# A fused attention and mixture-of-experts kernel: the scores of a later step move to between the two halves of the value mix on TensorE

## What is computed

```python
scores = scale * np.matmul(q, k.transpose(0, 1, 3, 2))
mask = (rel >= 0) & (rel < window)
scores = np.where(mask, scores + bias[None], -1000000000.0)
scores = scores - np.max(scores, axis=-1, keepdims=True)
attn = np.exp(scores)
attn = attn / (np.sum(attn, axis=-1, keepdims=True) + 1e-09)
x = np.matmul(attn, v)            # then reshaped to (2304, 512)
expert_idx = np.argmax(x @ w_gate, axis=1)
h = np.maximum(np.einsum('ecd,edf->ecf', disp, w1), 0.0)
y = np.einsum('ecf,efd->ecd', h, w2)
```

## Time and profile before

| what | value |
|---|---|
| median of 3 runs | 388.81 us (388.73 to 388.84) |
| the profiled execution, its own time | 388.75 us |
| span of the profile | 387.0 us |
| what lies around the span | 1.75 us |
| attention in the profile | about 11.4 to 135.8 us |
| TensorE busy | 370.0 us, 96% of the span |
| mean granted TensorE clock | 0.992 of full speed |

### The profile page before, as it was taken

One profiled execution on the slowest core, in us unless ns is written; L12 is line 12 of the kernel. 1 busy time (PEld: TensorE's weight loads), 2 busy tenths in 40 slices (PEclk: granted clock), 3 DMA queues, 4 the chain that ended last, 5 costly groups with the idle time before them and its releaser, 6 DMA issues.

```text
span 387.0 us, 8491 instructions
## 1 busy us (share of the span) xinstructions
PE 370.0 (96%) x2978; PEld 318.8 (82%) x2978; DVE 252.1 (65%) x798; ACT 202.2 (52%) x535; POOL 145.1 (37%) x192
## 2 busy tenths in 40 slices
PE   7999999998999998999999999999999999999990
PEld 6787778876877677989989989988989998989980
DVE  6788677799978763767966547556777775542120
ACT  2978878887777612664635424444637644411100
POOL 7558989945643342423042043034033240011011
PEclk9999999999999999999999999999999999999996
DMA  8999999999851111687687365664776666001001
GB/s 163 202 320 204 226 227 232 256 257 218 187 85 56 55 29 56 205 256 257 197 268 229 117 200 179 171 180 169 241 257 232 191 221 209 2 28 45 3 25 51
DMA packets 81326, 64.90 MB, mean 168 GB/s; under 512 B 63982, under 2 KB 63982, under 8 KB 81264
## 3 DMA queue, kind: packets, MB, share of 16 engines
q1 hardware_dynamic: 73600, 52.19, 51.0%
q0 software_dynamic: 3840, 11.03, 8.6%
q10 hardware_dynamic: 3824, 0.80, 1.2%
HBM read 54.56 MB, written 11.02 MB: 169 GB/s over the span
## 4 chain that ended last, share of the span: by engine, by line
PE 78%; POOL 10%; DVE 5%; issue 2%; DMA 2%; ACT 1%; SPq 1%; DVEq 0%; POOLq 0%
PE ps L1485 59%; PE ps L1343 4%; PE ps L1316 4%; POOL weights_sb L617 4%; PE ps L1354 3%; PE ps L1282 2%; PE ps L1478 2%; PE ps L1324 2%; DMA q_rows<-in_q 2%; POOL probsT L624 2%; POOL v_step L605 2%; POOL weights_sb L616 2%; DVE ps L907 1%; DVE probs L920 1%; PE ps L1400 0%
## 5 line engine op out<-in xcount | busy, mean ns | idle before, releaser
L1485 PE MATMUL ps<-weights_sb,hiddenT 128*128 128x512 f32 x480 | 118.5, 393 | 0.0
L1485 PE MATMUL ps<-rowsT_hi,weights_sb 128*128 128x256 f32 (+2 forms) x512 | 115.0, 303 | 1.0 <-DVE rowsT_lo L1163 1.0
L1485 PEld LDWEIGHTS ps<-weights_sb,hiddenT 128*128 128x128 f32 x480 | 87.6, 188 | 16.6 <-DVE hiddenT L1182 0.2
L857 ACT ACTIVATE hiddenT<-ps 128x384 fp32r<-128x384 f32 (+1 forms) x64 | 30.6, 478 | 111.8 <-PE ps L1485 111.6
L1485 PEld LDWEIGHTS ps<-rowsT_hi,weights_sb 128*128 128x128 f32 x512 | 85.8, 188 | 2.6 <-issue 1.4
L1190 DVE TENSOR_TENSOR weights_sb<-raw,weights_sb 128x1024 fp32r<-128x1024 f32 x56 | 68.4, 1222 | 17.1 <-ACT weights_sb L845 16.9
L1485 PE MATMUL ps<-rowsT_lo,weights_sb 128*128 128x256 f32 (+2 forms) x256 | 76.7, 300 | 0.0
L1182 DVE SCALAR_TENSOR_TENSOR hiddenT<-ps,hiddenT 128x384 fp32r<-128x384 f32 (+1 forms) x64 | 34.5, 539 | 56.0 <-ACT hiddenT L857 55.8
L845 ACT ACTIVATE weights_sb<-raw 128x1024 fp32r<-128x1024 f32 x56 | 58.9, 1052 | 0.0
L682 POOL DMA_INDIRECT gathered<-x_rows,src_row x21 | 23.1, 1098 | 91.9 <-DVE weight_now L1176 87.3
L743 ACT ACTIVATE probs<-probs,mins 128x128 f32<-128x128 f32 x144 | 55.6, 392 | 0.6 <-DVE mins L920 0.4
(11 more groups left out here) (175 smaller groups left out, 489.0 us busy)
## 6 DMA issues: line engine op xcount, KB each, us to landing
raw<-in_moe_w SPq DMA_DIRECT2D x64, 512.0 KB, 4.7
q_rows<-in_q SPq DMA_DIRECT2D x16, 256.0 KB, 5.9
v_rows<-in_v SPq DMA_DIRECT2D x16, 256.0 KB, 5.4
x_rows<-x_sb SPq DMA_DIRECT2D x16, 256.0 KB, 4.9
k_rows<-in_k SPq DMA_DIRECT2D x14, 256.0 KB, 6.3
k_rows<-in_k ACTq DMA_DIRECT2D x2, 256.0 KB, 7.0
v_rows<-in_v SPq DMA_DIRECT2D x4, 128.0 KB, 5.8
v_front<-in_v SPq DMA_DIRECT2D x4, 128.0 KB, 6.2
```

The costliest lines, as they stand in the source:

```text
L857: nc.scalar.activation(hiddenT[0][c % RINGED][:, 0:P * size], hiddenT_ps(c, P * size), ACT.Relu).then_inc(hiddenT_hi, 1)
L1485: ins = te.matmul(dst, left[a], right[c], start=first and n == 0, stop=last and n == 2)
```

## The change

`mix` gets a parameter for the half that it does. In a step, the first half (values as loaded) is issued before `score`, and the second half (differences) after it. The waits go with the halves: `v_landed` and `probsT_whole` ahead of the first, `v_stepped` and `probsT_later` ahead of the second. The waits for `first_kept` and `early_kept` move ahead of the first half, and so ahead of `score`. The first two steps of the first span keep their order. In the two steps that have no score left to issue nothing is moved. No instruction is added or taken away, and the queues of the other engines stay as they are.

```diff
-            def mix(b, kk):
+            def mix(b, kk, part):
 
                 i, quad = divmod(kk, 2)
                 u = b * TI + i
-                values = [v_rows[:, u % RING, :]] + ([v_step[:, u % 2, :]] if i > 0 else [])
-                if quad == 0:
-                    pe.wait_ge(v_landed[u % RING], landed(u))
-                pe.wait_ge(probsT_whole, b * STEPS + kk + 1)
...
+                final = part == (1 if i > 0 else 0)
+                if part == 0:
+                    if quad == 0:
+                        pe.wait_ge(v_landed[u % RING], landed(u))
+                    pe.wait_ge(probsT_whole, b * STEPS + kk + 1)
+                    left = v_rows[:, u % RING, :]
+                else:
+                    pe.wait_ge(v_stepped, b * (TI - 1) + i)
+                    pe.wait_ge(probsT_later, b * (STEPS - 2) + kk - 1)
+                    left = v_step[:, u % 2, :]
+                for n in range(2):
+                    for odd in range(2):
+                        h = head(quad, 2 * odd + n)
+                        last = te.matmul(mixT_ps[DH * odd:DH * odd + DH, n, :], left[:, DH * h:DH * h + DH],
+                                         probsT[:, part, 2 * odd + n, :], start=(part == 0), stop=final)
+                if final:
+                    last.then_inc(mixed, 1)
...
+                    if last and kk == FIRST_INVERTED:
+                        pe.wait_ge(first_kept, 1)
+                    if last and kk in (4, FIRST_ROUTED[1] + 4):
+                        pe.wait_ge(early_kept, 1 if kk == 4 else 3)
+                    if not first or i > 0:
+                        mix(b, kk, 0)
                     if not (last and kk + 2 >= STEPS):
                         if not first or kk >= 2:
                             pe.wait_ge(back_kept, b * STEPS + kk - 1)
                         score(b + (kk + 2) // STEPS, (kk + 2) % STEPS)
-                    if last and kk == FIRST_INVERTED:
-                        pe.wait_ge(first_kept, 1)
-                    if last and kk in (4, FIRST_ROUTED[1] + 4):
-                        pe.wait_ge(early_kept, 1 if kk == 4 else 3)
-                    mix(b, kk)
+                    if first and i == 0:
+                        mix(b, kk, 0)
+                    if i > 0:
+                        mix(b, kk, 1)
```

## The result

The changed kernel takes 403.26 us (median of 4 runs, 402.98 to 404.03) and the kernel before 388.77 us (4 runs, 388.71 to 388.84) on the same chip. The ratio is 1.0372, with a 95% interval of 1.036 to 1.0384: slower. The forecast was 401.6 us, in a range of 397.0 to 405.5. The profiled execution took 403.5 us, its span is 401.8.

A forecast was written before the change was run, and what follows sets the result against it. TensorE's queue bounds the kernel (busy 370.0 of 387.0 us). Terms: 7.5 - 1.4 + 0.6 + 2.35 + 3.7 = 12.8 us, so 388.75 + 12.8 = 401.55, stated as 401.6 us; range 397 to 405.5.

The forecast's parts named there:

- The wait on GpSimd: Second half of the mix waits for GpSimd's `keep_later` in six steps; the change gains all 1.4 us.
- The stall for ScalarE's copy: Between `turn_back` and first half, TensorE waits for the probabilities' copy: 0.32 us (0.27 to 0.41) in 32 steps.
- The extra change of tile shape: Halves of the mix split by the score cost 0.15 us more a step, in 30 steps; bounds 0 and 0.34.
- The rival in which it is free after a stall: Switch from first half to score hides in the stall: 3.9 us less, 397.7 us; chance 0.17.
- VectorE keeps up in normal steps: Between score and `turn_back`, `biased` takes about 2.16 us against 2.33 of other TensorE work: 0.17 us left.
- The rival that VectorE becomes the bound: `biased` comes later than 2.16 us and normal steps grow, 3.5 us more: 405.1 us; chance 0.15.
- The held steps: Span 2, steps 4, 10, 13: TensorE waits for VectorE's read; steps 4-6, 10-12, 13-15 cost 3.7 us more.
- The delay of `pick`: In steps 4, 10 and 13 of span 2, `pick` comes 1.26, 0.96 and 1.03 us later.
- from each, VectorE is busy without a gap: From `pick` to release of `turn_back` two steps on, VectorE has no idle time; the whole delay goes through.
- The held steps don't absorb their share: Rival judged: slack in VectorE's routing work absorbs the 3.7 us, leaving 9.1 more, 397.9 us; chance 0.08.
- The gain doesn't stand alone either: Rival judged: copy in time for first half, switch free, only the GpSimd wait goes: 387.4 us; chance 0.03.

The follow-up runs named there:

- experiments 2: Kernel before, with the turn of queries or keys issued behind `turn_probs` (late turn) and ScalarE's turned-query copy behind its probabilities copy: 390.42 us, ratio 1.0032.
- 6: Kernel before, TensorE's order untouched, first half of an odd step's weight split on GpSimd done in the even step before: 388.5 us, ratio 0.9989.
- experiment 1: Changed kernel, with the turn of queries or keys issued behind `turn_probs` and ScalarE's turned-query copy behind its probabilities copy: 399.28 us, ratio 1.026.
- experiment 7: Changed kernel, with both halves of the mix ahead of the score: 410.48 us, ratio 1.0552.
- Experiment 3: Changed kernel, with the old order (score, wait, both halves) in steps 4, 10 and 13 of span 2 only: 398.65 us, ratio 1.0238.
- experiment 4: Changed kernel, with GpSimd's `v_step` of step 5 of span 2 held back until VectorE's keys are done: 402.3 us, ratio 1.0337.
- experiment 5: Kernel before, with the turn behind `turn_probs` and ScalarE's turned-query copy behind its probabilities copy in steps 2 to 17 of span 1 alone: 387.62 us, ratio 0.9974.

## Why the prediction was right, point by point

- **The wait on GpSimd** The earlier trace rows is gone as forecast. That it was worth 1.4 us is shown without the change: experiments 2 and 6 take 1.41 and 1.33 us out of steps 4 to 17 of span 1.
- **The stall for ScalarE's copy** was put at 0.32 us a step. It is 0.34 (3.84 less the 3.50 of experiment 1), and the two kinds of step stand at the two ends of the forecast 0.27 to 0.41: `turn_back` to first half, less 0.58, is 0.27 in odd and 0.42 in even ones. In the odd steps the way from the copy's end (62.25) to the first half (62.30) is 0.05 us, as in the earlier trace rows. In the even ones it is 0.15 (66.06 to 66.21): there the upper bound, taken from GpSimd, was nearer. The 0.32 for all steps comes close because it lies between the two.
- **The extra change of tile shape** was put at 0.15 a step, and the new order costs 0.15 beyond the stall (experiments 1 and 2). The rival in which it is free after a stall is ruled out for normal steps, since score follows the first half by 0.58 us behind a stall and by 0.59 without one. The Trainium skill, TensorEngine Tiling (Array Packing), Key Properties, says that changing the mode drains the engine; experiments 1 and 2 agree with it, and put 0.15 us on it in this order.
- **VectorE keeps up in normal steps.** The first pair of minima ends at 64.99 (64.91 and 0.08), `turn_back` starts at 65.21: 0.22, less the 0.06 of the way, is 0.16, against 0.17 forecast. The rival that VectorE becomes the bound didn't come about in the changed kernel. How thin the 0.17 is, experiment 1 shows in span 2 and experiment 7 throughout.
- **The held steps** were the term that was mis-sized: 4.45 us instead of 3.7. Experiment 3 shows that the new order in steps 4, 10 and 13, with the score behind the moved waits, is the cause of all of it. The delay of `pick` was right in sum: from `turn_probs` to `pick` it grew by 1.04, 0.76 and 1.25 us, 3.05 in all, for 3.25. The single ones, forecast at 1.26, 0.96 and 1.03, miss by 0.20 to 0.22 either way and partly cancel, which is luck: VectorE's reads didn't stay where they were, but ended 0.20 and 0.19 us earlier in steps 4 and 10 and 0.24 later in step 13, counted from `turn_probs`. What failed was the step "from each, VectorE is busy without a gap", taken to mean that its work keeps its length. In steps 5 and 14 the delay brought small operations of VectorE beside other work of GpSimd. Beyond the delays and the 0.15 for the split, the three groups took 0.56, 0.02 and 0.37 us more. In step 5 `key` took 1.21 us instead of 0.60 and `past` 0.38 instead of 0.17, while `sums_eps` took 0.16 instead of 0.41: together 0.57. In step 14 `past` took 0.53 instead of 0.17, 0.36 more. For the first, experiment 4 moved GpSimd's operation and with it most of the cost (0.50); for the second nothing was tried. The delay also shows one step sooner than the prediction had it: at 102.85 us, at the end of step 5, TensorE's turn of the queries waits 0.83 us for VectorE's copy of the keys (line 930).
- **What else is in the total.** The excess of 1.41 us (14.21 for 12.8) is 0.75 here, 0.28 in span 1, where the mean step is 3.84 for 3.82, 0.08 in the three other lines of the table, and 0.31 ahead of the first step that the change touches. The last is no part of the change: experiments 3 and 4 have the changed kernel's order there and reach kk = 2 at 18.37 and 17.84 us, experiment 6 has the old order and 18.16. From the start of the experts to the end the profiled execution takes another 0.59 us more (251.83 for 251.24); in the seven experiments it is 251.22 to 251.49, so this looks like scatter too.
- **The rivals.** The held steps don't absorb their share: with the old order in three of them experiment 3 gives 4.58 us back in the nine steps, for the 3.7 booked. The gain doesn't stand alone either: the copy is late in every normal step. Experiment 1, without that stall, starts the experts 4.45 us earlier. That is less than the 23 x 0.32 = 7.4 booked for the stall, because in span 2 the late turn brings out waits for VectorE instead.

## What to carry to other kernels

Moving a piece of work on the busiest engine to win 0.2 us at one wait also moves what it covered: list, for each group that now stands earlier, what releases it and when that is done, and for each that stands later, who is queued behind it. A gain may be had without the cost by moving another piece: here the turn, in span 1 alone, where VectorE has slack (experiment 5, 0.26%). In span 2 the same move costs more than it brings (experiments 1 and 2). Where an engine near its bound is delayed as a block, look also at what its small operations will then run beside.

## What the runs showed of the hardware

Operations of VectorE on a few columns can take as long as GpSimd's 128x512 operation beside them. A sum of two 128x8 tiles in SBUF (`sums_eps`) takes 0.15 us at its shortest and took 1.29 beside a subtraction of 1.27 that started with it, 0.69 where it came in the middle of one. Their ends fall together each time (77.14 and 77.11; 102.00 and 101.97 us). The Trainium skill, SBUF — State Buffer, Who interferes with whom, states this as a rule: an operation of VectorE with two inputs in SBUF and one of GpSimd that reads SBUF exclude each other for the whole instruction. The traces agree. The copies of 128x512 from PSUM beside the same GpSimd operation keep their 0.69 us (100.70 in experiment 4).

TensorE doesn't always start equally soon behind the same engine: in the changed kernel the way from the end of ScalarE's copy to the first half is 0.05 us in odd steps and 0.14 to 0.15 in even ones. What makes the difference wasn't tried.
